# mLSTM, soft mixture and SoLU layer on one core: the product P kept in PSUM, the exponents' second part fetched per tile, and TensorE's steps in another order

## The reference

```python
for t in range(S):
    m_new = np.maximum(f_gate[:, :, t] + m, i_gate[:, :, t])
    f_stab = np.exp(f_gate[:, :, t] + m - m_new)
    i_stab = np.exp(i_gate[:, :, t] - m_new)
    m = m_new
    C = f_stab[:, :, None, None] * C + i_stab[:, :, None, None] * np.einsum('bhd,bhe->bhde', vt, kt)
    n = f_stab[:, :, None] * n + i_stab[:, :, None] * kt
    h_tilde = np.einsum('bhde,bhe->bhd', C, qt)
    denom = np.maximum(np.abs(nq), 1.0)        # nq = n . q
    y[:, :, t] = o * h_tilde / denom           # o = sigmoid(o_gate)
```

## Time and profile before

| | |
|---|---|
| median of 3 runs | 331.17 us (328.66 to 331.35) |
| profiled execution, its own time | 331.48 us |
| its span, first to last instruction | 329.3 us |
| mean granted TensorE clock | 0.964 |
| PE busy / DVE busy / ACT busy / POOL busy | 276.9 / 256.8 / 144.4 / 174.3 us |
| time from 0 to 22 us | gates turned into rows on DVE, inputs loaded |
| 22 to 57 us | tiles 0 to 3 |
| 57 to 148 us | tiles 4 to 19, a steady pattern |
| 148 to 177 us | tiles 20 to 23 and the drain |
| 177 to 329 us | mixture and SoLU layer |

### The profile page before, as it was taken

How to read it: one execution, slowest core, us unless ns; L and a number is a source line. 1 busy time by engine, 2 the same in 40 slices (tenths; PEclk the granted TensorE clock), 3 DMA queues, 4 the chain that set the end, 5 groups by cost and what they waited for, 6 DMA issues and landing times. The chain is left out here.

```text
span 329.3 us, 8741 instructions
## 1 busy us (share of the span) xinstructions
PE 276.9 (84%) x3311; PEld 202.9 (62%) x3345; DVE 256.8 (78%) x419; ACT 144.4 (44%) x222; POOL 174.3 (53%) x334
## 2 busy tenths in 40 slices
PE   0028999999999999999984898487499999999996
PEld 0025788888888888888872325131166666666664
DVE  8964669999999999998754459213999999999951
ACT  1453012232323222232321073401998888888850
POOL 3602245655556465554540029410688888888880
PEclk9999999999999999999995699989789999999999
DMA  7960038767766865744004999600379999998993
GB/s 236 352 239 0 2 83 282 224 198 262 263 187 206 291 238 170 265 128 116 2 2 145 349 407 430 266 2 0 76 148 171 197 170 212 156 211 189 179 209 106
DMA packets 64553, 60.68 MB, mean 184 GB/s; under 512 B 52800, under 2 KB 56896, under 8 KB 61952
## 3 DMA queue, kind: packets, MB, share of 16 engines
q1 hardware_dynamic: 64512, 60.12, 64.4%
HBM read 43.59 MB, written 3.93 MB: 144 GB/s over the span
## 5 line engine op out<-in xcount | busy, mean ns | idle before, releaser
L904 DVE TENSOR_TENSOR arena<-arena 128x512 bf16<-128x512 f32 x48 | 64.9, 1351 | 0.0
L797 ACT ACTIVATE arena<-ps 128x512 f32<-128x512 f32 x48 | 28.7, 598 | 68.1 <-PE ps L546 68.1
L774 PE MATMUL ps<-wouth,ring 128*128 128x320 bf16 x192 | 54.3, 306 | 1.4 <-DMA ring<-ring 0.9
L775 PE MATMUL ps<-woutl,ring 128*128 128x320 bf16 x192 | 54.2, 305 | 0.0
L896 DVE TENSOR_TENSOR arena<-ps,arena 128x512 f32<-128x512 f32 x48 | 32.9, 686 | 10.9 <-ACT arena L797 8.2
L434 POOL TENSOR_TENSOR arena<-arena 128x328 f32<-128x328 f32 x20 | 15.0, 751 | 45.9 <-ACT arena L797 45.9
L1125 DVE TENSOR_REDUCE ring<-ps 128x1 f32<-128x1024 f32 x24 | 29.2, 1222 | 5.6 <-PE ps L765 5.4
L879 ACT ACTIVATE ring<-ring 128x1024 bf16<-128x1024 f32 x24 | 27.6, 1149 | 10.4 <-POOL ring L527 10.4
L560 PE MATMUL ps<-arena 40*128 40x128 f32 x384 | 30.6, 304 | 1.7 <-DVE arena L896 1.7
L778 PE MATMUL ps<-wouth,ring 128*128 128x320 bf16 x192 | 30.0, 299 | 0.0
L543 PE MATMUL ps<-causal,identb 128*128 128x512 bf16 x25 | 10.6, 424 | 22.3 <-DVE arena L1006 22.3
(11 more groups left out here) (174 smaller groups left out, 689.9 us busy)
## 6 DMA issues: line engine op xcount, KB each, us to landing
ring<-w_dram SPq DMA_DIRECT2D x10, 1280.0 KB, 8.9
arena<-kv_dram SPq DMA_DIRECT2D x24, 324.0 KB, 4.6
arena<-qkT_dram SPq DMA_DIRECT2D x48, 160.0 KB
sig<-o_gate_dram SPq DMA_DIRECT2D x3, 1280.0 KB, 11.4
arena<-w_dram SPq DMA_DIRECT2D x3, 1280.0 KB, 8.8
sig<-w_dram SPq DMA_DIRECT2D x3, 1280.0 KB, 9.6
out_dram<-ring SPq DMA_DIRECT2D x24, 160.0 KB, 2.2
arena<-w_out_dram SPq DMA_DIRECT2D x1, 1280.0 KB, 6.2
```

Source lines behind the costliest of these rows:

```text
L774: pe.matmul(o, UHT[i % 4][:, j, :], wouth[:, j, :], start=(j == 0), stop=False)
L775: pe.matmul(o, UHT[i % 4][:, j, :], woutl[:, j, :], start=False, stop=False)
L797: act.activation(WT[i % 2][:, hf * HALF * L:(hf + 1) * HALF * L], bE, ACT.Exp).then_inc(s["w_ready"], 1)
L904: dve.tensor_tensor(low(pf), pf, high(pf), ALU.subtract).then_inc(s["pl_ready"], 1)
```

## The change

P is multiplied in place in PSUM (bS to bS). ACT, which had no part in this, rounds it into a bf16 tile PH (`p_high`), and DVE subtracts PH from bS into a bf16 tile PL. The four products of selector and L3 in `exponents` go. In their place the three bf16 parts of L are written once to a DRAM tensor `kept` and, tile by tile, 3 x 8 x 128 values of it are fetched into three partitions below the 96 of the selector; three rows of ones stand below A3, so that one product with 99 rows gives a_s + L_t. The calls in the steps of PE, ACT and DVE are in another order. `scores(n)` now waits for `pl_ready` of the tile before, since bS is held until the subtraction has read it.

```diff
+            def load_row(i):
+                c, b = i // B, i % B
+                sp.dma_start(pick[G3:GL, b * H:(b + 1) * H, :],
+                             kept.rearrange("(r h) t -> r h t", r=3)[:, b * H:(b + 1) * H, c * L:(c + 1) * L]) \
+                    .then_inc(l_in[b], 16)
             load_tile(2)
             load_tile(3)
+            sp.wait_ge(s["l_ready"], 1)
+            sp.dma_start(kept, L3[0:G3, :]).then_inc(s["l_kept"], 16)
+            sp.wait_ge(s["l_kept"], 16)
+            for i in range(B):
+                load_row(i)
...
             for i in range(B, NT):
+                sp.wait_ge(s["e_done"], 2 * (i - B) + 2)
+                load_row(i)
...
 PE exponents:
+                pe.wait_ge(l_in[b], 16 * (c + 1))
                 pe.matmul(bE, identb[:, :], causal[:, :], start=True, stop=False)
-                pe.matmul(bE, A3[0:G3, c * L:(c + 1) * L], pick[:, head:head + HALF, :], start=False, stop=False)
-                for j in range(HALF):
-                    last = pe.matmul(bE[:, j * L:(j + 1) * L], pick[:, head + j, :], L3[0:G3, c * L:(c + 1) * L],
-                                     start=False, stop=(j == HALF - 1))
+                last = pe.matmul(bE, A3[0:GL, c * L:(c + 1) * L], pick[0:GL, head:head + HALF, :], start=False, stop=True)
 PE scores:
-                await_(pe, "p_ready", 2 * i)
+                await_(pe, "pl_ready", 2 * i)
 PE logits:
-                await_(pe, "state_ready", min(n - 1, NT - B))
+                await_(pe, "state_ready", min(n, NT - B))
 PE step:
                 exponents(n, 0)
-                scores(n)
-                exponents(n, 1)
                 if n == 0:
                     coefficients()
+                add_to_state(n)
+                transpose_x(n)
+                exponents(n, 1)
+                scores(n)
                 weigh_values(n)
                 logits(n)
-                add_to_state(n)
-                transpose_x(n)
 ACT:
+            def p_high(n, hf):
...
+                act.wait_ge(s["p_ready"], 2 * i + hf + 1)
+                await_(act, "o_done", i - 1)
+                act.copy(PH[i % 2][:, cols], bS[hf]).then_inc(s["ph_ready"], 1)
             def step(n):
                 weights_of(n, 0)
+                copy_xt(n)
                 weights_of(n, 1)
-                copy_xt(n)
+                p_high(n, 0)
+                p_high(n, 1)
 DVE:
-                await_(dve, "o_done", i - 1)
-                dve.tensor_tensor(PF[i % 2][:, cols], bS[hf], WT[i % 2][:, cols], ALU.mult).then_inc(s["p_ready"], 1)
+                dve.tensor_tensor(bS[hf], bS[hf], WT[i % 2][:, cols], ALU.mult).then_inc(s["p_ready"], 1)
...
-                dve.tensor_tensor(low(pf), pf, high(pf), ALU.subtract).then_inc(s["pl_ready"], 1)
+                dve.wait_ge(s["ph_ready"], 2 * i + hf + 1)
+                await_(dve, "o_done", i - 1)
+                dve.tensor_tensor(PL[i % 2][:, cols], bS[hf], PH[i % 2][:, cols], ALU.subtract).then_inc(s["pl_ready"], 1)
...
+            dve.memset(A3[G3:GL, :], 1.0)
...
             def step(n):
-                p_product(n, 0)
                 if n == 0:
                     copy_coefficients()
+                add_state(n)
+                p_product(n, 0)
+                p_product(n, 1)
                 scale_inter(n)
                 p_low(n, 0)
-                p_product(n, 1)
+                p_low(n, 1)
                 sum_up(n)
-                p_low(n, 1)
                 denominator(n)
                 invert(n)
-                add_state(n)
                 copy_logits(n)
```

More of the change, by code:

```diff
@@ L12, with mlstm_softmoe_solu @@
 P = 128
-def mlstm_softmoe_solu(nc, qkT, kv1, o_gate, f_gate, i_gate, phi, w1, w2, w_in, w_out, g_ln, out, dims):
+def mlstm_softmoe_solu(nc, kept, qkT, kv1, o_gate, f_gate, i_gate, phi, w1, w2, w_in, w_out, g_ln, out, dims):
     B, H, S, D, E, SLOTS, F = dims
@@ L45, in mlstm_softmoe_solu @@
     G3 = 3 * BH
+    GL = G3 + 3
     HB = F // 2
@@ L62, in mlstm_softmoe_solu @@
         pick_words = sb("pick_words", [P, BH * L // 2], F32)
-        pick = pick_words[:, :].bitcast(BF16).rearrange("p (h t) -> p h t", h=BH)[0:G3]
+        pick = pick_words[:, :].bitcast(BF16).rearrange("p (h t) -> p h t", h=BH)
         lo_rows_g = sb("lo_rows_g", [P, 1], F32)
@@ L106, in mlstm_softmoe_solu @@
         WT = [carve(H * L) for _ in range(2)]
-        PF = [carve(H * L) for _ in range(2)]
+        PH = [carve(H * L, BF16) for _ in range(2)]
+        PL = [carve(H * L, BF16) for _ in range(2)]
         inter = [carve(H * HV) for _ in range(2)]
@@ L189, in mlstm_softmoe_solu @@
         gates_in phi_in gcol_in pool_step consts_ready ident_ready ident_copied dve_const m_ready im_ready ll_ready
[L190 removed]
+        row_step coef_rows coef_exp rows_ready l_ready l_kept
         coefT_done gammaP_done coefs_ready
         v_ready s_done e_done w_ready i_done i_scaled
[L193 removed]
+        p_ready ph_ready pl_ready o_done num_ready den_ready rden8_ready scaled_ready sig_ready y_ready
         vd_ready x_done decayed state_ready xt_done xt_copied lg_done lg_ready
@@ L203, in mlstm_softmoe_solu @@
         qk_in = [ctx.enter_context(nc.semaphore(f"qk_in{b}")) for b in range(B)]
+        l_in = [ctx.enter_context(nc.semaphore(f"l_in{b}")) for b in range(B)]
         kv_in = [ctx.enter_context(nc.semaphore(f"kv_in{b}")) for b in range(B)]
@@ L584, in weigh_values @@
                     vh, vl = high(values_of(b)[:, cols]), VL[b][:, cols]
-                    p = PF[i % 2][:, h * L:(h + 1) * L]
-                    ph, pl = high(p), low(p)
+                    ph, pl = (p[i % 2][:, h * L:(h + 1) * L] for p in (PH, PL))
                     pe.matmul(bO[:, cols], ph, vh, start=True, stop=False)
@@ L805, in copy_xt @@
                 act.copy(XT[i % 2].rearrange("p k t -> p (k t)"), bM[:, 0:NP * P]).then_inc(s["xt_copied"], 1)
+            def p_high(n, hf):
+                i = tile_at(n, 0)
+                if i is None:
+                    return
+                cols = slice(hf * HALF * L, (hf + 1) * HALF * L)
+                act.wait_ge(s["p_ready"], 2 * i + hf + 1)
+                await_(act, "o_done", i - 1)
+                act.copy(PH[i % 2][:, cols], bS[hf]).then_inc(s["ph_ready"], 1)
             def step(n):
                 weights_of(n, 0)
+                copy_xt(n)
                 weights_of(n, 1)
-                copy_xt(n)
+                p_high(n, 0)
+                p_high(n, 1)
             act.wait_ge(s["pool_step"], 1)
@@ L975, in _ @@
             dve.wait_ge(s["dve_const"], 2)
-            dve.tensor_copy(pick, again(own_row[:, :], 2, L)).then_inc(s["consts_ready"], 1)
+            dve.tensor_copy(pick[0:G3], again(own_row[:, :], 2, L)).then_inc(s["consts_ready"], 1)
             dve.wait_ge(s["gates_in"], 32)
@@ L999, in _ @@
             dve.tensor_copy(L3[BH:2 * BH, :], high(rest_l))
-            dve.tensor_tensor(L3[2 * BH:3 * BH, :], rest_l, high(rest_l), ALU.subtract)
+            dve.tensor_tensor(L3[2 * BH:3 * BH, :], rest_l, high(rest_l), ALU.subtract).then_inc(s["l_ready"], 1)
             dve.wait_ge(s["im_ready"], 1)
@@ L1197 @@
     out = nc.dram_tensor("out_dram", (NC * B, P, DM), F32, kind="ExternalOutput").ap()
-    mlstm_softmoe_solu(nc, *args, out, (B, H, S, D, E, SLOTS, F))
+    kept = nc.dram_tensor("kept_dram", (3 * B * H, S), BF16, kind="Internal").ap()
+    mlstm_softmoe_solu(nc, kept, *args, out, (B, H, S, D, E, SLOTS, F))
     r = run_bass_kernel_spmd(nc, [{f"{n}_dram": a for n, a in arrays.items()}], core_ids=[0])
```

3 lines of the change are left out of this document (1 added, 2 removed).

## The result

The changed kernel takes 370.3 us (median of 4 runs, 365.7 to 371.2) against 331.26: a ratio of 1.117 (95% interval 1.108 to 1.126). The profiled execution took 370.34 us, with a span of 368.6 against 329.3. All runs are of one core; in what follows, the runs of some experiments lie far apart because their TensorE clock did, so ranges stand beside the medians, and ratios are of the runs near the fastest.

The account below looks back on a forecast made before the run. PE was taken as the bound at 5.70 us a step, DVE right behind. The terms summed as 331.48 + 13.4 + 0.2 - 2.9 + 2.5 = 344.7 us, so 344.5 for the median; range 337 to 358.

Parts of the forecast that it names:

- R3: Rival: holes in PE's step lower its clock; six steps at 1.2 GHz give 360 us, all 395; chance 0.13.
- main case: Sum of the terms, 344.7 us; step between 6.35 and 6.95 us, time 339 to 354; chance 0.75.
- (d): Steady step: PE waits 1.26 us at add_to_state for the logits' copy; loop 6.54 us against 5.70, +13.4 us.
- (a): Exponents on PE: four small products less save 0.21 us in each half, 0.42 us a step, 5.70 to 5.28.
- (b): DVE: low parts from PSUM and products into PSUM take 0.69 us each; DVE's work a step becomes about 3.9 us.
- (c): ACT's rounding: two operations out of PSUM a step, like the exponential's 0.60 us; ACT has room for them.
- R4: Rival: one low part on DVE stays at 2.25 us; step 8.1 us, time 370 us; chance 0.04.
- (e): Tiles 20 to 23: no add_to_state wait, but 0.6 us for the first exponential; three steps 16.1 us, +0.2 us.
- (f): Drain after tile 23's first product: transposes ahead of logits, copy beside them; -2.9 us, bounds -3.5 and -1.
- (g): Start: the first fetched row lands at 27.0 us, tile 1's first product at 39.0; +2.5 us, bounds 0 and +8.
- R1: Rival: PE is not held at add_to_state and its own work sets the step; 324.6 us; chance 0.04.
- R2: Rival: DVE's chain is shorter by about 0.7 us; step 5.8 us, time 331 to 334 us; chance 0.04.

Follow-up runs that it names:

- run 10: Kernel before with only the new order of calls, P in SBUF and the four products kept: 402.33 us (392.7 to 410.5).
- run 1: Changed kernel with unused matmuls on PE before add_to_state in steps 5 to 23, filling the hole: 347.56 us, ratio 1.052.
- run 4: Changed kernel with the logits in another PSUM bank, so add_to_state need not wait for their copy: median 333.4 us over ten runs, ratio 0.997.
- run 6: Kernel before with the exponents' change alone (fetched rows, one product with 99 rows): 323.23 us, ratio 0.978.
- run 7: Kernel before with P in PSUM and ACT's rounding alone, old order and exponents: 333.47 us over ten runs, ratio 1.011.
- Run 9: Exponents' change alone with early row fetches, plus transposes ahead of logits from step 24 on: 320.12 us, ratio 0.964.
- run 2: Changed kernel with the logits' copy earlier on DVE, right behind the second low part: median 353.5 us, 337.1 to 376.2.
- run 3: All the changed kernel's parts with the calls in the order of the kernel before: four runs, 332.5, 337.6, 405.7, 408.8 us.
- run 11: Repeat of the changed kernel's parts in the old order, twelve runs: three at 405 to 407 us, nine at 330 to 337, ratio 1.003.
- run 8: Exponents' change alone, with the copy to DRAM and two row fetches ahead of the loads of tiles 2 and 3: 321.09 us, ratio 0.963.
- run 5: Changed kernel with logits in another bank, plus the mask product done twice in each half's exponents: 340.56 us, ratio 1.030.
- run 12: Changed kernel's parts in the old order, plus the mask product done twice: six runs at 336.4 to 340.3 us, ratio 1.023.

## Why the prediction was wrong, by its steps

**What failed is the weight of R3, the clock**: the sum of the main case left the clock at its high level, a term put at nothing, and R3 got 0.13. Its sentence was "the clock stays at 1.00 where PE has few holes, and the hole here is a single short one". A single hole of 1.3 us in a step of 6.7 us was enough: the clock fell in the fifth such step, in run 10 as well, which cost about 24 of the 39 us, and filling the hole removed all but one short fall (run 1) and 23 us. The rule of the Trainium skill ("TensorE: Matmul & The Clock Gate", A second HAM failure mode: psum-queue depth-cycling) agrees with the windows above: 1.00, 0.50 from 85 to 126 us, 1.00, 0.50 from about 171. R3's own prices, 360 us for six steps at the low level and 395 for all, bracket the result, and its 9.1 us for such a step was 9.35. The text's own sign of being wrong, matmuls at double length in the steady stretch, is what showed.

**(d) was right in place, cause and nearly in size.** Predicted: hole 1.26 us, loop 6.54. Measured: 1.33 and 6.68. Nearly all of the difference is in one term: from the copy's start to add_to_state's first matmul it is 0.40 us where I had 0.28. The copy started at t+3.65, where I had t+3.64. I had given the copy 0.18 us; rows 5 show 0.15, and so does the trace after, which changes nothing in the start. Moving the logits away (run 4) took 37 us off.

**The main case's number is that of run 1.** With the clock held, the changed kernel's profiled execution took 346.27 us; I had 344.7. That they lie so close is in part luck. By the same stretches as in the table, run 1 has -1.8 us at the start where I had +2.5, +17.7 over the 16 steps (one of them, the first filled one, 8.46 us long) for +13.4, +0.1 for +0.2 in tiles 20 to 23, and -0.5 for -2.9 in the drain; the errors of the terms, up to 4.3 us, largely cancel.

**(a)**, 0.42 us a step: right, 5.29 to 5.30 us in run 6 against a computed 5.28. **(b)**: products 0.695 and low parts 0.680 for 0.69 each; hardly any price for writing to PSUM shows. What the Trainium skill ("ScalarE: Activation LUTs", Step-by-step: what each stage is for) says of VectorE lying closer to SBUF shows as 9 ns here: 695 ns into PSUM (699 in run 7, in the old order), 686 into SBUF. **(c)**: 585 ns, hidden. R4 is out by the same rows; that its price, 370 us, is the time measured is chance, since no low part was slow and the step that it had at 8.1 us was 6.68 or 9.35.

**(e) and (f)** were sized at the high level and ran at the low one: +10.5 and +0.6 for +0.2 and -2.9. Run 9 shows the drain's gain when the clock is up, at most 2.4 us.

**(g)** was wrong in sign though right in its parts: rows landed at 28.2 (I had 27.0), tile 1's first product came at 40.17 (39.0), but the clock rose earlier than before (the first scores of 1.16 us start at 44.94, where before it was 49.73) and tile 4 was reached 1.4 us sooner, not 2.5 later. The place where the clock rises was in my text as a cost only.

**R1 and R2** did not happen: at the high level nothing but the named wait decided.

**What stays open** is why the kernels that have both P in PSUM and the removed products (runs 2, 3, 4, 11) have single executions with the clock low for most of the attention, while the exponents alone, with the same queue on PE as runs 3 and 11, had none in sixteen executions (runs 6, 8, 9). What differs in PE's steps is what the scores wait for. Either half alone is not enough: with the columns gone and P in SBUF there were none of sixteen, with P in PSUM and the columns kept or put back in another form (runs 5, 7, 12) none of twenty, and with both, leaving out run 2, which has a hole, six of twenty-six near 400 us. So neither the columns alone nor the scores' wait alone fits these counts, and how the two would work together is not shown. No trace of an execution near 406 us was taken, so whether the clock fell or never rose there is not shown.

## What to carry to other kernels

When calls are reordered, follow each wait that stays in the code with a step number in it: `n - 4` meant a copy a whole step old in one order and the copy just ahead in the other, and it put DVE's full chain in series with PE. Price a hole on TensorE twice, once for its length and once for the clock, even if it is short and comes once per step; a filler that nobody reads shows in one run how much of the time is the hole's length and how much the clock. And try the parts of a change one by one: here one part was worth 2%, and 3 to 4% with its DMAs ahead of the bulk loads, one gained nothing (1% slower), and one, the order, cost some 70 us alone.

## What the runs showed of the hardware

- One hole of 1.3 to 1.4 us per 6.7 to 7.2 us step took the granted clock from 1.00 to 0.50 in the fifth such step (the changed kernel and run 10; in the seventh the second time), with PE otherwise at work, and work at 0.50 without holes (20.00 of 20 us busy in the window shown) did not bring it back for over 100 us in run 10, while in the changed kernel it came back after 41 us. Holes of 0.51 us did the same in the profiled execution of run 2, in the sixth such step and, after each return to 1.00, in the second. So no count of steps follows from these traces. Before the change PE also ran its first matmuls at the 1.2 GHz level, from 22.27 us on: the scores take 2.08 us at 23.64 us and 1.16 us for the first time at 49.73.
- The same kernel on the same inputs took 330 or 406 us (run 11), with mean clocks of 0.958 and 0.735.
- DVE's product with the result in PSUM takes 695 ns, in SBUF 686 ns. A subtraction with one operand in PSUM takes 680 ns beside POOL's work, where one with both operands in SBUF took 2.25 us.
